# Attention, gated FFN and expert layer on one core: the softmax division is moved behind the PV product, and the split of the FFN weights is moved to GpSimd

## What is computed

```python
# q, k, v: (4, 8, 576, 64) fp32; block = 64
scores = q @ k.T / 8;  scores[block_i < block_j] = -1e9      # block-causal mask
attn = exp(scores - max);  attn = attn / (sum(attn) + 1e-9)
x = (attn @ v) as (2304, 512)
h = sigmoid(x @ w_gate) * (x @ w_val)                        # d_ff 1536
y = h @ w_out
# then top-1 of 8 experts: relu(y @ w1[e]) @ w2[e], times its gate probability
```

## Time and profile before

| | |
|---|---|
| three timed runs | 1021.36, 1023.47, 1024.10 us (median 1023.47) |
| span of the profiled execution | 1022.1 us |
| TensorE busy | 948.0 us (93%), weight loads 783.2 us (77%) |
| VectorE, ScalarE, GpSimd busy | 594.7 (58%), 338.1 (33%), 244.4 us (24%) |
| attention, first S(0) to the first FFN matmul | 6.97 to 246.08 us |
| FFN stage, share of TensorE that is busy from 250 to 700 us | all of it (450.0 of 450 us) |
| mean granted TensorE clock | 0.969 of full speed |
| granted clock, 236 to 244 us (behind the last stall of attention) | 0.95, then 0.50 |

### The profile page before, as it was taken

One profiled execution on the slowest core, in us unless ns is written; L12 is line 12 of the kernel. 1 busy time (PEld: TensorE's weight loads), 2 busy tenths in 40 slices (PEclk: granted clock), 3 DMA queues, 4 the chain that ended last, 5 costly groups with the idle time before them and its releaser, 6 DMA issues.

```text
span 1022.1 us, 15500 instructions
## 1 busy us (share of the span) xinstructions
PE 948.0 (93%) x5050; PEld 783.2 (77%) x5051; DVE 594.7 (58%) x1106; ACT 338.1 (33%) x772; POOL 244.4 (24%) x241
## 2 busy tenths in 40 slices
PE   6888889888999999999999999999468998999995
PEld 3555545556999999999999999999457886888884
DVE  6878787785776555565565555555654444225421
ACT  4656666654222121211211221211153344114410
POOL 2122122121121111111111111111163535125421
PEclk9999999998999999999999999999779998999998
DMA  4234434331211010000010000000265537115310
GB/s 123 72 100 125 122 91 123 112 115 60 83 42 42 31 31 1 32 31 1 32 31 1 31 1 1 32 1 1 110 223 181 201 122 272 41 41 205 128 41 29
DMA packets 57315, 78.30 MB, mean 77 GB/s; under 512 B 22703, under 2 KB 34991, under 8 KB 57264
## 3 DMA queue, kind: packets, MB, share of 16 engines
q1 hardware_dynamic: 51504, 62.42, 19.5%
q0 software_dynamic: 3360, 10.49, 2.9%
q10 hardware_dynamic: 2400, 4.72, 1.2%
HBM read 63.46 MB, written 14.68 MB: 76 GB/s over the span
## 4 chain that ended last, share of the span: by engine, by line
PE 82%; DVE 7%; issue 5%; DMA 2%; POOL 2%; ACT 1%; SPq 0%; DVEq 0%; POOLq 0%; ACTq 0%
PE bank L1161 21%; PE bank L1163 21%; PE bank L1162 21%; PE bank L1092 6%; PE bank L1129 5%; PE bank L1111 3%; DVE prob L817 3%; PE bank L1298 2%; DMA stage<-in_we 1%; PE bank L1220 1%; DVE nmax L836 1%; PE bank L1272 1%; POOL ew1l L368 1%; PE bank L1211 1%; DVE pt L314 1%
## 5 line engine op out<-in xcount | busy, mean ns | idle before, releaser
L1161 PE MATMUL bank<-xh,w1h 128*128 128x384 f32 x576 | 196.1, 340 | 0.1
L1163 PE MATMUL bank<-xh,w1l 128*128 128x384 f32 x576 | 193.2, 335 | 0.0
L1162 PE MATMUL bank<-xl,w1h 128*128 128x384 f32 x576 | 193.1, 335 | 0.0
L888 DVE RECIPROCAL sig<-egate 128x384 f32<-128x384 f32 x72 | 183.8, 2553 | 2.5
L550 POOL TENSOR_TENSOR hl<-hraw,hh 128x384 fp32r<-128x384 f32 x72 | 78.2, 1085 | 401.7 <-ACT hh L696 401.7
L885 DVE TENSOR_SCALAR egate<-egate 128x384 f32<-128x384 f32 x72 | 27.5, 382 | 190.0 <-ACT egate L725 190.0
L1092 PE MATMUL bank<-kt,qbd 128*128 128x512 f32 (+7 forms) x320 | 116.6, 459 | 7.0 <-DVE kt L799 7.0
L696 ACT CAST hh<-hraw 128x384 fp32r<-128x384 f32 x72 | 37.0, 514 | 229.9 <-DVE hraw L893 226.3
L1161 PEld LDWEIGHTS bank<-xh,w1h 128*128 128x128 f32 x576 | 108.3, 188 | 2.2 <-DVE hraw L893 0.4
L1162 PEld LDWEIGHTS bank<-xl,w1h 128*128 128x128 f32 x576 | 108.3, 188 | 1.7
L1163 PEld LDWEIGHTS bank<-xh,w1l 128*128 128x128 f32 x576 | 108.1, 188 | 0.0
(11 more groups left out here) (150 smaller groups left out, 1524.4 us busy)
## 6 DMA issues: line engine op xcount, KB each, us to landing
stage<-in_we SPq DMA_DIRECT2D x56, 512.0 KB, 4.2
w1raw<-in_w SPq DMA_DIRECT2D x8, 768.0 KB, 4.4
kt<-in_kT SPq DMA_DIRECT2D x16, 288.0 KB, 3.3
qbd<-in_qT SPq DMA_DIRECT2D x32, 144.0 KB, 3.8
xt_scratch<-xo SPq DMA_DIRECT2D x16, 288.0 KB, 2.1
xraw<-xt_scratch SPq DMA_DIRECT2D x6, 768.0 KB, 4.6
y_scratch<-yrow ACTq DMA_DIRECT2D x6, 768.0 KB, 3.5
vt<-in_v SPq DMA_DIRECT2D x16, 256.0 KB, 2.8
```

What stands on the lines that cost most here:

```text
L888: dve.reciprocal(sig[:], egate[:, f % 2, :]).then_inc(sig_done, 1)
L1161: pe.matmul(out_, wh, ah, start=first, stop=False, skip_group_check=True)
L1162: pe.matmul(out_, wh, al, start=False, stop=False, skip_group_check=True)
L1163: return pe.matmul(out_, wl, ah, start=False, stop=last, skip_group_check=True)
```

## The change

The probabilities are no longer divided before they are transposed. `prob` gets a place for each of the nine blocks, padded with zeros to whole tiles, and T(j) always transposes tiles of 128 x 128. After all nine sums of a pair are known, VectorE makes all nine reciprocals at once (`recips`, in its step 2 of the next pair). GpSimd spreads them over a matrix `dmat` (`dmat_of`: a stacked identity times the reciprocals, 128 x 576), and two matmuls of TensorE with a block of ones (`rwide_of`, steps 6 and 7) broadcast them over the partitions, half a pair at a time through one half of bank 2. ScalarE copies each half to `rwide` (`rwide_out`, its steps 6 and 7), and VectorE multiplies the PV output with it into `xo` (`o_out`, its step 8). ScalarE's copies to `xo` go. The evacuation of u3, u5, u6 and u8 goes from ScalarE to VectorE, and that of u7 and u9 from VectorE to ScalarE. The cast to `w1h` goes from ScalarE to GpSimd, ahead of the subtraction and behind `dmat_of`. PV is cut at column 288 instead of 320.

```diff
-        BY_ACT = {1, 3, 5, 6, 8}
+        BY_ACT = {1, 7, 9}
...
-        def pT_psum(u):
-            return bank[2][:, u % 2, :]
-        O_CUT = 5
+        O_CUT = S // 2
+        PT_BANK = {0: 0, 1: 1, 2: 0, 3: 1, 4: 1, 5: 1, 6: 0, 7: 1, 8: 0, 9: 1}
+        BEFORE = {0: 8, 1: 9, 2: 0, 3: 1, 4: 3, 5: 4, 6: 2, 7: 5, 8: 6, 9: 7}
+        def rwide_psum(half):
+            return bank[2][:, 0, 0:O_CUT]
...
-        W1_STEP = [4, 5, 6]
+        RWIDE_STEP = {6: 0, 7: 1}
+        RSUM_STEP, O_STEP = 2, 8
...
-            def w1_low_half(k):
-                pool.wait_ge(w1_high, W1_PARTS * (k + 1))
+            def w1_split(k):
+                pool.wait_ge(w1_loaded, 16 * (k + 1))
+                pool.tensor_copy(w1h[:, bass.ds(k, 1), :].rearrange("p a f -> p (a f)"), w1raw[:]).then_inc(w1_high, 1)
+                pool.wait_ge(w1_high, k + 1)
                 pool.tensor_tensor(w1l[:, bass.ds(k, 1), :].rearrange("p a f -> p (a f)"), w1raw[:],
...
+            def dmat_of(g, par):
+                pool.wait_ge(rinv_done, g + 1)
...
+                pool.tensor_tensor(dmat[:], istack[:].unsqueeze(1).to_broadcast(D3),
+                                   rinv[:, par, :].unsqueeze(2).to_broadcast(D3), ALU.mult).then_inc(dmat_done, 1)
...
                     pool.tensor_scalar(kt[p % 2][:], kt[p % 2][:], SCALE, None, ALU.mult).then_inc(kt_scaled, 1)
 
+                if not (isinstance(g, int) and g == 0):
+                    dmat_of(g - 1, (p - 1) % 2)
                 if p == 2:
-                    w1_low_half(2 * b)
+                    w1_split(2 * b)
                 elif p == 0 and not isinstance(b, int):
-                    w1_low_half(2 * b - 1)
+                    w1_split(2 * b - 1)
...
+            def rwide_out(g, half):
+                act.wait_ge(rwide_mm, 2 * g + half + 1)
...
+                act.copy(rwide[:, half, :], rwide_psum(half)).then_inc(rwide_done, 1)
...
-                    if i == O_STEP and not start:
-                        o_out(g - 1, p - 1)
+                    if i in RWIDE_STEP and not start:
+                        rwide_out(g - 1, RWIDE_STEP[i])
...
+            def recips(g, par):
+                dve.wait_ge(exp_done, NB * (g + 1))
+                dve.tensor_scalar(rsum1[:], rsum[:, par, :], 1e-9, None, ALU.add).then_inc(rsum1_done, 1)
...
+                dve.reciprocal(rinv[:, par, :], rsum1[:]).then_inc(rinv_done, 1)
+            def o_out(g, par):
+                dve.wait_ge(pv_done, g + 1)
+                dve.wait_ge(rwide_done, 2 * g + 2)
...
+                dve.tensor_tensor(xo[par][:].rearrange("p (a n) -> p a n", a=2), rwide[:], bank[3][:, :, 0:O_CUT],
+                                  ALU.mult).then_inc(xo_done, 1)
...
-                    if not (start and i < 2):
-                        recip(n - 2, (s - 2) % SLOTS)
+                    if i == RSUM_STEP and not start:
+                        recips(g - 1, (p - 1) % 2)
                     if i >= LAG:
                         after_unit(g, p, i - LAG)
                     elif not start:
                         after_unit(g - 1, p - 1, i + NB - LAG)
-                    if not (start and i < 2):
-                        norm(n - 2, (i - 2) % NB, (s - 2) % SLOTS)
-                    if not (start and i < 1):
-                        denominator(n - 1, (s - 1) % SLOTS)
+                    if i == O_STEP and not start:
+                        o_out(g - 1, (p - 1) % 2)
...
-                pe.wait_ge(norm_done, NB * g + j + 1)
+                pe.wait_ge(exp_done, NB * g + j + 1)
...
+            def rwide_of(g, half, u):
+                if half == 0:
+                    pe.wait_ge(dmat_done, g + 1)
...
+                    out_by(*u)
+                else:
+                    pe.wait_ge(rwide_done, 2 * g + 1)
+                pe.matmul(rwide_psum(half), hones[:],
+                          dmat[:].rearrange("p i q -> p (i q)")[:, half * O_CUT:(half + 1) * O_CUT],
+                          start=True, stop=True).then_inc(rwide_mm, 1)
...
                         turn(g - 1, p - 1, i + NB - PE_LAG)
+                    if i in RWIDE_STEP and not start:
+                        rwide_of(g - 1, RWIDE_STEP[i], (2, g))
                     if i in PV_STEP and not start:
                         pv(g - 1, p - 1, PV_STEP[i])
...
             pv(NPAIR - 1, PPB - 1, list(range(KT_N)))
+            rwide_of(NPAIR - 1, 0, (8, NPAIR - 1))
+            rwide_of(NPAIR - 1, 1, None)
```

More of the change, by code:

```diff
@@ L103, in bass_attention_ffn_moe @@
         vt = [sb(s1, f"vt{i}", [P, KT_N, P]) for i in range(2)]
-        prob = sb(s1, "prob", [P, SLOTS, S])
-        pt = [sb(s1, f"pt{i}", [P, KT_N, NB, P]) for i in range(2)]
+        prob = sb(s1, "prob", [P, P * sum(i // 2 + 1 for i in range(NB))])
+        pt = [sb(s1, f"pt{i}", [P, PT_STEP * (KT_N - 1) + 2 * S]) for i in range(2)]
         xo = [sb(s1, f"xo{i}", [P, S]) for i in range(2)]
[L107 to L110, removed]
+        nmax = sb(s1, "nmax", [P, NB])
+        rsum = sb(s1, "rsum", [P, 2, NB])
+        rsum1 = sb(s1, "rsum1", [P, NB])
+        rinv = sb(s1, "rinv", [P, 2, NB])
+        istack = sb(s1, "istack", [P, BLK])
+        hones = sb(s1, "hones", [P, P])
+        dmat = sb(s1, "dmat", [P, NB, BLK])
+        rwide = sb(s1, "rwide", [P, 2, S // 2])
         s1.close()
@@ L287, in scores_at, with oT_at @@
             return bank[o // 2][:].rearrange("p a n -> p (a n)")[:, 0:S]
-        def pT_psum(u):
-            return bank[2][:, u % 2, :]
-        O_CUT = 5
[L294 to L297, removed]
+        O_CUT = S // 2
+        def oT_at(h, a, e):
+            half = a // O_CUT
+            return bank[3][64 * h:64 * h + 64, half, a - half * O_CUT:e - half * O_CUT]
+        PT_BANK = {0: 0, 1: 1, 2: 0, 3: 1, 4: 1, 5: 1, 6: 0, 7: 1, 8: 0, 9: 1}
+        BEFORE = {0: 8, 1: 9, 2: 0, 3: 1, 4: 3, 5: 4, 6: 2, 7: 5, 8: 6, 9: 7}
+        def pT_psum(u):
+            return bank[2][:, PT_BANK[u], :]
+        def rwide_psum(half):
+            return bank[2][:, 0, 0:O_CUT]
+        prob_at = {}
+        for j in range(NB):
+            prob_at[j] = sum(P * tiles_of(x) for x in ORDER[:j])
         LAG, PE_LAG = 3, 4
-        W1_STEP = [4, 5, 6]
-        W1_PARTS = len(W1_STEP)
+        W1_STEP = 4
         PV_STEP = {4: [0], 5: [1], 6: [2], 7: [3, 4]}
-        O_STEP = 8
+        RWIDE_STEP = {6: 0, 7: 1}
+        RSUM_STEP, O_STEP = 2, 8
         def evac_pT(copy, p, j, u, t0, t1, done):
             i = ORDER[j]
[L310 to L318, removed]
+            rows = pt[p % 2][:]
+            copy(bass.AP(tensor=rows.tensor, offset=rows.offset + PT_STEP * t0 + BLK * i,
+                         ap=[rows.ap[0], [PT_STEP, t1 - t0], [S, 2], [1, BLK]]),
+                 pT_psum(u)[:, 0:(t1 - t0) * P].rearrange("p (t h q) -> p t h q", h=2, q=BLK)).then_inc(done, 1)
         def gv_psum(f):
@@ L639, in after_unit @@
                         evac_pT(act.copy, p, j, u, t0, t1, pT_out_a)
[L641 to L648, removed]
+            def rwide_out(g, half):
+                act.wait_ge(rwide_mm, 2 * g + half + 1)
+                if half == 0 and not (isinstance(g, int) and g == 0):
+                    act.wait_ge(xo_done, g)
+                act.copy(rwide[:, half, :], rwide_psum(half)).then_inc(rwide_done, 1)
             def pair(b, p):
@@ L654, in pair @@
                     n = NB * g + i
-                    s = (NB * p + i) % SLOTS
                     act.wait_ge(nmax_done, n + 1)
[L657 to L660, removed]
+                    if not start:
+                        act.wait_ge(pT_done, NU * (g - 1) + i + 2)
+                    act.activation(prob[:, prob_at[i]:prob_at[i] + width(i)], scores_at(p, i), ACT.Exp,
+                                   bias=nmax[:, i:i + 1], accum_out=rsum[:, p % 2, ORDER[i]:ORDER[i] + 1]
+                                   ).then_inc(exp_done, 1)
                     if i >= LAG:
@@ L687, in _ @@
             xhigh(0, 0)
-            o_out(NPAIR - 1, 1)
+            rwide_out(NPAIR - 1, 0)
+            rwide_out(NPAIR - 1, 1)
             act.wait_ge(scores_done, NB * NPAIR)
@@ L867, in _ @@
             xlow(0, 0)
+            o_out(NPAIR - 1, 1)
             def yT_evac(i, m, last=False):
```

102 lines of the change are left out of this document (52 added, 50 removed).

## The result

The changed kernel takes 1026.07 us (median of 8 runs, 1024.36 to 1028.95), the kernel before 1023.82 (8 runs beside it, 1021.36 to 1024.96). The ratio is 1.0026, with a 95% interval of 1.0015 to 1.0038: slower by 2.3 us, where 10 us were forecast. The interval leaves out 1, but the difference is less than the 3 us that the prediction named as what can be told from no change.

What follows compares the result with a forecast made beforehand. TensorE, busy 93% of the span, was taken as the bound, with norm stalls in attention. Pairs +33.9, first pair -0.7, stalls -20.9, tail -2.1 sum to +10.2 us: 1033.5 us forecast, range 1022 to 1043.

Steps and rivals of the forecast that it cites:

- both new waits: TensorE in each pair: S(3) waits for exp(0'), +0.61 us; second broadcast waits for ScalarE's copy, +1.65 with its work.
- The removed stall: Attention: VectorE's norm, held by GpSimd's subtraction in every second pair, goes; 7 stalls of 2.99 us, -20.9 us.
- rival 5: Attention: an evacuation or `o_out` meets GpSimd's longer work as norm did, 3 us in 7 pairs, 1054 us; chance 0.05.
- The added time of a pair: Attention: two new waits and broadcast work on TensorE, +0.61 and +1.65 us, lengthen a pair from 13.04 to 15.30 us.
- the first chain: u6's copy and `o_out` on VectorE delay max(0'), exp(0') and so S(3) on TensorE: +0.61 us per pair.
- the second: u3's copy, max(6), exp(6) and ScalarE's copy hold the second broadcast 0.45 us: +1.65 us per pair, 1.20 of it work.
- rival 2: One new wait absent or half as long because VectorE is less late: 1025 to 1027 us; chance 0.17.
- The start-up: Start of pair 0, left as it is; its waits for norm may give up to 1 us, not in the sum.
- The tail: Last T(4)'s issue to first FFN matmul: 8.9 us instead of 11.0 at full clock, -2.1 us; nothing at half clock.
- What was at nothing: Terms taken as free: recut PV and unchanged number of transposes on TensorE, and removal of ScalarE's casts in steps 4 to 6.
- the rival with the late keys: GpSimd's cast delays scaling of the next pair's keys, which S(0') needs: up to +9 us, 1043 us; chance 0.15.
- The rival by which TensorE alone bounds the pair: Attention: TensorE's own work of 13.2 us sets the pair, attention ends 20 us early, 1003 us; chance 0.13.

Runs made afterwards that it cites:

- e4: The kernel before, with GpSimd's subtraction cut to 96 of 1536 columns of each piece: 1007.28 us, ratio 0.9832.
- e5: The kernel before, whole computation, with the subtraction moved from GpSimd to VectorE in three parts: 1002.38 us, ratio 0.9786.
- e9: The changed kernel with `o_out` behind max(0'), first broadcast copy ahead of exp(6), u8's copy on ScalarE, u9's on VectorE, and fp32r broadcast: 1004.45 us, ratio 0.981.
- e7: The changed kernel with the cast to `w1h` back on ScalarE in three parts: 1029.35 us, ratio 1.0048.
- e8: The changed kernel with `o_out` behind max(0'), first broadcast copy ahead of exp(6), u8's copy on ScalarE and u9's on VectorE: 1010.90 us, ratio 0.9879.
- e1: The changed kernel with `o_out` moved on VectorE from ahead of max(0') to right behind it: 1026.91 us, ratio 1.0023.
- e2: The changed kernel with ScalarE's copy of the first broadcast half moved ahead of exp(6): 1018.88 us, ratio 0.9945.

## Why the prediction was right and wrong

The direction was right, and both new waits were at their places; the size was over four times too large. All of it lies in attention. Measured at the same marks:

| stretch | forecast | measured |
|---|---|---|
| start of the trace to the first PV0 | -0.1 | -1.95 (24.41 to 22.46) |
| 14 pairs from there | +10.7 | +5.3 (203.47 to 208.76) |
| last PV0 of a full pair to the first FFN matmul | -0.4 | -1.5 (18.2 to 16.7) |
| sum | +10.2 | +1.8 |

Of the 8.4 us between the two sums, 5.4 lie in the pairs, 1.9 in the start-up and 1.1 in the tail.

**The removed stall** was right: -20.9 forecast, and e4 has 20.5 less over the same pairs. That norm waits as long as the subtraction runs, and nothing else makes the long pairs, is shown by e4 and e5. That `o_out` doesn't take norm's place (rival 5) is shown by its row beside the last subtraction.

**The added time of a pair was mis-sized, and this is the step that failed**: 2.26 us forecast, 14.91 - 13.07 = 1.84 measured. The terms that were wrong are the hand-overs between engines. "S(3) starts 0.22 later, as at 137.94": in the earlier trace rows S(3) follows T(7), which starts at 137.59 and is issued in 0.35, so TensorE was busy until then and the 0.22 was no wake-up. After the change exp(0')'s sum is read at 124.61 and S(3) starts at 124.67: 0.06. I used the 0.22 twice (the second broadcast starts 0.05 behind its copy), and 0.1 for ScalarE's wake-up, which is 0.03 for exp(6) (131.50 + 0.55 to 132.08) and 0.04 for exp(0') in most pairs (0.12 in the one shown). In the first chain this makes the difference between +0.61 and +0.42 us (PV0 to S(0') is 8.65 us, so S(0') to PV0 6.26 on the mean), in the second between +1.65 and +1.45. The other links hold to 0.1 us: max(0') at +2.45 (forecast +2.46), `o_out` 0.74 (0.75), the copy of 288 columns 0.39 (0.40); u3's copy starts 0.20 behind the end of T(2) (0.11), and exp(6) takes 0.57 until ScalarE's copy starts (0.67), which nearly cancel. Times 14 pairs the two errors are 5.5 us.

**The measured time is that of rival 2** (1025 to 1027), and its condition is half met: the second broadcast waits 0.22 us (0.42 behind T(3), less 0.20 of issue) where 0.45 were forecast. But its reason, that VectorE would be less late, is not what happened; VectorE is late as worked out. The hit on the number is in part luck, as the start-up and the tail gave 3 us that this rival did not have.

**The start-up** I had left as it is. Its gaps for norm gave 1.2 us (first S(0) to first PV0 17.4 before, 16.2 after), a little over the 1 us that I named and did not put into the sum; 0.7 more is that the first S(0) came at 6.26 instead of 6.97, because the first loads landed earlier in this execution.

**The tail** came out 0.9 us shorter than worked out (8.05 from T(4)'s issue, 8.9 forecast): the last PV at full clock takes 3.1 us where I had added its parts to 3.5, and the two broadcasts with the copy 1.6 where I had 2.0. That the clock is full there was an assumption, which the prediction named; e9's tail shows that it need not be.

**What was at nothing** was so by the rows, though no run changed it alone: from PV0 to the next score matmul it is 1.13 us before and after, and from PV2 to S(7) 0.70 and 0.75. That ScalarE's casts cost the pairs nothing is shown by 13 of e7's 14. GpSimd's cast took 1.46 us (2.3 taken) and `dmat` 1.15 (1.75), so there were 2 us of slack against the rival with the late keys; e9 shows such a wait where pairs are 13 us, with loads and not the cast as its cause. The estimated 2.3 us by the Trainium skill (GPSIMD Engine Reference, section 3.1) was too high as well. The rival by which TensorE alone bounds the pair was not there in the change, and e8 and e9 show what it took: three moves for 13.8 us, and the cheaper broadcast for 13.1 in most pairs. (The chances named for slower, same and faster are off by 0.02 at most: 0.5, 0.15, 0.05 and a third of 0.17 make 0.76, not 0.74.)

**What I had not seen**: that the wait of S(3) had a second chain beside it, almost as long, so that taking `o_out` out of the first was worth nothing by itself (e1). The forecast of the pair was not hurt by that, a forecast of e1 was.

So the change takes 20.5 us of stall away, adds 25.8 us over the same 14 pairs (about 1.2 us of new work on TensorE per pair, the rest waits), and gains 3.5 us at the ends. The cheaper cure, e5, takes the stall away and adds almost nothing.

## What to carry to other kernels

When one engine's long instruction holds another's, move or shorten that instruction before rebuilding the algorithm around it: the rebuilt one bought 20 us and paid 26 in matmuls and waits. When evacuations and side work are handed to the engine that feeds the critical chain (here VectorE's copies ahead of its maxima), the idle share of that engine says nothing; count what stands ahead of the first link of the next tile, and look for a second chain of the same length before moving one link. And take a hand-over time only from a row in which the waiting engine was really idle.

## What the runs showed of the hardware

- A GpSimd memset, which reads nothing, held a VectorE scalar multiply from SBUF to SBUF for 7.1 us (7.58 instead of 0.46, in e4).
- Two subtractions that both read two operands from SBUF overlap in their records, but by their ends the second waited for the first. In e7's tail GpSimd's was first and took its usual 3.44 us; VectorE's ended 1.62 us behind it (249.66 to 251.28). In the tail of the changed kernel VectorE's took 2.41 us (1.76 before) and ended 1.62 us behind GpSimd's cast (245.17 to 246.79); GpSimd's subtraction took 4.86 (3.44 elsewhere) and ended 3.32 us behind VectorE's (250.11). First VectorE's row, then GpSimd's:

```profile
244.38 2.41 DVE L880 TENSOR_TENSOR xl<-xraw,xh 128x1536 fp32r<-128x1536 f32 x1 [1.56 <-ACT xh L702]
```

```profile
245.25 4.86 POOL L536 TENSOR_TENSOR w1l<-w1raw,w1h 128x1536 fp32r<-128x1536 f32 x1
```

- Not every GpSimd instruction holds VectorE until its end. In the kernel before, norm of 448 columns ran inside the scaling of the keys and took no longer than elsewhere (0.44 us at 233.68), while the scaling took 1.82 us instead of 1.65; norm of 512 columns at 129.41 took 0.79 instead of 0.47 under another, and ended 0.70 before it. First GpSimd's row, then VectorE's:

```profile
145.32 1.82 POOL L531 TENSOR_SCALAR kt<-kt 128x576 f32<-128x576 f32 x1 [14.42 <-DMA qbd<-in_qT]
```

```profile
146.18 0.45 DVE L817 TENSOR_SCALAR prob<-prob,rinv 128x448 f32<-128x448 f32 x1
```

- On GpSimd a cast of 1536 columns (1.46 us) is faster than a scalar multiply of 576 (1.65 us).
- An idle of 0.15 us on TensorE was worth 0.41 us when it was taken away (e2).
